# Attention on Trainium2: queries of a later head turned right behind the last key tile of the next head, and the pieces of the maxima behind them placed one behind each score

## What is computed

```python
q_pool = q.reshape(B, H, S // 2, 2, D).mean(axis=3)       # B 4, H 8, S 1152, D 64
scores = scale * np.matmul(q_pool, k.transpose(0, 1, 3, 2))
scores = scores - np.max(scores, axis=-1, keepdims=True)
attn = np.exp(scores)
attn = attn / (np.sum(attn, axis=-1, keepdims=True) + 1e-09)
return np.matmul(attn, v)
```

## Time and profile before

| | |
|---|---|
| median of 3 runs | 1168.25 us |
| the profiled execution's own time | 1168.3 us |
| its span, from first to last instruction | 1166.5 us |
| around the span | 1.8 us |
| mean granted TensorE clock | 0.992 of full speed |
| attention | from the start to about 500 us |
| PE busy | 1118.7 us, 96% of the span |
| DVE, POOL, ACT busy | 807.6, 689.0 and 620.7 us |

### The profile page before, as it was taken

One profiled execution on the slowest core, in us unless ns is written; L12 is line 12 of the kernel. 1 busy time (PEld: TensorE's weight loads), 2 busy tenths in 40 slices (PEclk: granted clock), 3 DMA queues, 4 the chain that ended last, 5 costly groups with the idle time before them and its releaser, 6 DMA issues. The chain is left out here.

```text
span 1166.5 us, 19903 instructions
## 1 busy us (share of the span) xinstructions
PE 1118.7 (96%) x7088; PEld 928.8 (80%) x7088; DVE 807.6 (69%) x1573; ACT 620.7 (53%) x1228; POOL 689.0 (59%) x694
## 2 busy tenths in 40 slices
PE   6999999999999999997998989889999999999998
PEld 5777788777877778786877777668888888888897
DVE  5788888888888888866556555675548764685554
ACT  4666666666666666546565656643334333433331
POOL 5899999998899899834333335532254333632330
PEclk9999999999999999998999999999999999999999
DMA  8211122222221111000001002332112521233121
GB/s 209 62 54 47 55 63 62 62 62 62 62 62 55 45 56 41 22 13 25 1 1 41 2 26 71 105 104 72 50 60 73 181 57 53 72 90 103 53 63 55
DMA packets 76593, 71.47 MB, mean 61 GB/s; under 512 B 11856, under 2 KB 54864, under 8 KB 76496
## 3 DMA queue, kind: packets, MB, share of 16 engines
q1 hardware_dynamic: 75888, 69.90, 19.8%
q10 hardware_dynamic: 608, 0.30, 0.1%
HBM read 60.74 MB, written 9.44 MB: 60 GB/s over the span
## 5 line engine op out<-in xcount | busy, mean ns | idle before, releaser
L653 DVE TENSOR_REDUCE part_max<-psA 128x1 f32<-128x384 f32 x465 | 250.5, 556 | 55.5 <-PE psA L388 31.9
L582 ACT ACTIVATE pT<-psA 128x576 f32<-128x576 f32 x288 | 187.8, 652 | 154.0 <-PE psA L407 144.2
L279 POOL TENSOR_TENSOR pT<-pT 128x576 f32<-128x576 f32 x157 | 222.6, 1418 | 24.0 <-ACT pT L582 1.5
L2177 DVE TENSOR_TENSOR hidden_parts<-psC,hidden_parts 128x384 f32<-128x384 f32 x168 | 91.0, 554 | 123.5 <-PE psC L2024 121.5
L388 PE MATMUL psA<-kT,qT 128*128 128x384 f32 x465 | 165.7, 378 | 1.1 <-DVE part_max L653 0.6
L421 PE MATMUL psA<-pT,v_raw 128*64 128x288 f32 x1152 | 153.8, 412 | 0.0
L1848 POOL TENSOR_TENSOR w_raw<-w_raw 128x256 f32<-128x256 f32 x24 | 18.1, 756 | 206.8 <-DMA w_raw<-in_moe_w_ch 206.6
L398 PE MATMUL psA<-qT,kT 128*128 128x288 f32 x576 | 132.3, 311 | 0.0
L407 PE MATMUL psA<-qTm,kT 128*128 128x288 f32 x576 | 123.3, 296 | 0.5 <-ACT qTm L568 0.5
L421 PEld LDWEIGHTS psA<-pT,v_raw 128*64 128x64 f32 x1152 | 77.0, 136 | 53.2 <-issue 6.4
L398 PEld LDWEIGHTS psA<-qT,kT 128*128 128x128 f32 x576 | 98.6, 189 | 18.3 <-issue 14.0
(11 more groups left out here) (196 smaller groups left out, 2631.2 us busy)
## 6 DMA issues: line engine op xcount, KB each, us to landing
w_raw<-in_moe_w_ch SPq DMA_DIRECT2D x48, 256.0 KB, 3.1
k_raw<-in_k SPq DMA_DIRECT2D x32, 288.0 KB, 3.2
v_raw<-in_v SPq DMA_DIRECT2D x32, 288.0 KB, 2.8
q_raw<-in_q SPq DMA_DIRECT2D x31, 256.0 KB, 3.3
w_even<-in_moe_w_ch SPq DMA_DIRECT2D x12, 512.0 KB, 5.0
w_odd<-in_moe_w_ch SPq DMA_DIRECT2D x12, 512.0 KB, 4.8
u_rows<-x_all SPq DMA_DIRECT2D x16, 256.0 KB, 2.0
u_even<-u_rows SPq DMA_DIRECT2D x2, 1536.0 KB, 6.8
```

The source lines that it names most:

```text
L279: nc.gpsimd.tensor_tensor(pT[:, KT, :], pT[:, KT, :], pT[:, j, :], ALU.add).then_inc(part_summed, 1)
L582: nc.scalar.activation(pT[:, j, :].rearrange("p (a c) -> p a c", a=2), scores[n % 2][:, :, 0:HALF], ACT.Exp, scale=0.5 * float(D) ** -0.5) ...
L653: nc.vector.tensor_reduce(part_max[u][:, t, c:c + 1], maxes[n % 2][:, 0:PIECE], AX.X, ALU.max).then_inc(max_freed[n % 2], 1)
L2177: nc.vector.tensor_tensor(to, session((k, n))[:, 0:W], other, ALU.add).then_inc(added, 1)
```

## The change

On PE, `turn_queries(h + 2)` moves from behind m3 to right behind the "kc" lot of head h + 1. From there on m2 goes ahead of s1 and m3 ahead of s2, where they stood behind s1 and s2. The order from s3 on is as it was. On ACT the copy of the turned queries moves from behind e2 to right behind the copies of "kc", so ahead of e1. No instruction is added, taken away or resized.

```diff
                 score(h, 0)
                 maxima(0, 2)
                 turn_keys(h + 1, "kc", [KT - 1])
-                score(h, 1)
-                maxima(2, 3)
-                score(h, 2)
-                maxima(3, 4)
                 if more2:
                     turn_queries(h + 2)
+                maxima(2, 3)
+                score(h, 1)
+                maxima(3, 4)
+                score(h, 2)
                 maxima(4, 5)
                 score(h, 3)
                 maxima(5, 6)
...
                     exponent(h, j)
                     if j == 0:
                         copy_keys(h + 1, "kc")
-                    if j == 2 and more2:
-                        copy_queries(h + 2)
+                        if more2:
+                            copy_queries(h + 2)
                     if j == 5 and more2:
                         copy_keys(h + 2, "ka")
```

## The result

The changed kernel takes 1176.56 us in the median of 5 runs (1175.32 to 1179.6), the kernel before 1168.27 us (5 runs, 1167.49 to 1171.03). The ratio is 1.0072, 95% interval 1.0056 to 1.0089: 8.3 us slower. The forecast was 1177.4, with a range of 1172.3 to 1181.0.

A forecast was written before the change was run, and what follows sets the result against it. PE and DVE were taken to bound each other by handing over pieces of the maxima. Heads 1 to 29 at 0.30 us (8.7) and head 30 at 0.36, together 9.1, on 1168.3 gave 1177.4 us; range 1172.3 to 1181.0.

The forecast's parts named there:

- m2's place: PE, top of a head: m2's weight load starts 0.05 us behind m0's reduction in either order; s1 follows m2 by 0.28.
- Three scores between m2 and m5: PE: three scores replace two scores and the transposes between m2 and m5, making m5 0.16 us later a head.
- s3 waits for e1: PE: s3 needs the score buffer e1 reads, is released at 317.68, m5 starts at 318.31; bounds nothing and 0.29 us.
- The weight load behind a waiting piece: PE, s1 behind waiting m2: its load isn't made ahead, so 0.28 us is kept; otherwise some 0.10 a head lower.
- The copy of the queries at nothing: ACT, ahead of e1: the 0.59 us copy ends 0.2 us before e1's scores are there, so it costs nothing.
- the one I priced at 0.15: Rival on ACT: transposes or copy last longer, e1 a further 0.15 us late, 0.45 a head, 1182.3 us; chance 0.06.
- Nothing given back: PE and DVE behind m5: m7 and all that follows move with m5, and no place returns the time.
- The sum: Whole attention: heads 1 to 29 lose 29 x 0.30 = 8.7 us, with head 30 together 9.1 us.
- Head 0, put at nothing: First head, running at its own start-up pace: left at no loss; one head weighs 0.3 us either way.
- the 0.36 of the forecast: Head 30, without transposes to lose: m5 would stand 2.33 us behind m2's release, not 1.97, 0.36 us more.
- lowest corner: PE: smallest loss if only the order costs, 0.06 us a head, given as 1170.5 us.
- order alone: Rival on PE: 0.16 us a head, no wait for e1 or s1's load pulled ahead, 1173.3 us; chance 0.16.

The follow-up runs named there:

- its control: Kernel before, with the exponent of tile 1 computed for the first 288 of 576 queries in heads 1 to 30: 1167.68 us, ratio 0.9992.
- second-half kernel: Kernel before with s4 ahead of m7, row sums between m7 and m8, and later pieces, scores and turn of ka rewoven: 1164.98 us, ratio 0.998.

## Why the prediction was right

Forecast 1177.4, measured 1176.56; forecast 9.1 us of loss, measured 8.3, and 8.8 in the attention of the profiled execution. By its own steps:

- *m2's place.* Forecast: 0.05 behind the end of m0's reduction in either order, s1 another 0.28 behind. Measured 0.05 and 0.28. The run with only the pieces moved shows the same place with nothing in front of it.
- *Three scores between m2 and m5.* Forecast 0.16 a head. Measured 0.15: with e1 shortened the changed kernel is at 15.49, against 15.34.
- *s3 waits for e1.* Forecast 0.13 to 0.14. Measured 0.13, by the shortened exponent and its control. This was the step that hung on 0.05 us of reckoning, and it held.
- *The weight load behind a waiting piece.* The row at m7 said that it isn't made ahead, and in the changed kernel it isn't either: s1's load starts at 321.25, 0.11 behind m2's own load (321.14), which is the one that waits, and s1 follows m2 by 0.28. The Trainium skill (TensorE: Matmul & The Clock Gate, Step-by-step: what each phase is for) speaks of weight loads that are pulled ahead of matmuls in flight. This trace doesn't contradict that; it shows that no load was made ahead of a piece that still waited.
- *The copy of the queries at nothing.* It ends at 321.84, e1 starts at 322.14, and putting it back changes nothing. Where it was in the way, with PE's old order, it cost 1.26 us a head (16.60 against 15.34). That is a later turn than the one I priced at 0.15, so that price wasn't tested.
- *Nothing given back.* m7's whole delay reaches the next head, but for some 0.02: forecast distance 15.64, measured 15.63 between the first and last head of the even part. The profile shows no other return.
- *The sum.* 9.1 against 8.3 by the medians is within what the runs scatter (the interval of the ratio is 6.5 to 10.4 us); by the attention alone it is 9.1 against 8.8. That this is so near is in part luck. By the distances of single heads, heads 1 to 29 cost 8.1 and not 8.7. Head 0, put at nothing, cost 0.27 (its distance went from 14.92 to 15.19). Head 30 cost 0.37, against the 0.36 of the forecast (15.72 to 16.09). Together that is 8.7; the 8.8 comes from rounded starts.
- *A slip.* The lowest corner of the rival "order alone" at 0.06 a head is 31 x 0.06 = 1.9 us, so 1170.2 and not 1170.5. Nothing hangs on it.

One number came out wrong behind the prediction: the expectation of the run with the early turn alone had 0.02 to 0.08 us a head, and it costs 0.21, for a score behind transposes is longer than I reckoned and m4 takes over the stop of m2. The prediction's own rows had the hint: there m4 and s3 behind the transposes took 0.77 and not 0.70. So three of the four ways to place these two things are slower than the kernel before, two with a stop at m2 and one with a stop at m4.

## What to carry to other kernels

Where two engines hand two buffers to and fro, a piece can't start before a fixed time behind the piece two places before it. Count what stands between such a pair: work that fits exactly is hidden, and less of it leaves a stop that everything queued behind it pays for. Here a short job (the transposes) took the place of a long one (a score), and the stop was the difference. An independent long job in front of a piece that waits takes the stop away, as s4 in front of m7 showed. Then look for the next release that becomes late: here it was an exponent in the changed kernel, and the other engine's sums in the kernels with s4 moved.

## What the runs showed of the hardware that I had not expected

- A wait that was fulfilled long ago isn't free on PE when the instruction stands first in the queue: m4 with two waits started 0.12 us behind the reduction that released it, with one wait 0.05.
- A score behind transposes takes 0.60 us until the next piece starts, one behind a piece 0.52. In the run with the early turn alone its second matmul starts 0.20 behind its first, where it is 0.13 in a score behind a piece. That its weight loads set the pace there is likely and not shown.
- DVE's first sum of the exponents (L674), the same instruction in every kernel, has no fixed length. In the second-half kernel over the even part (least, median and most in ns):

```profile
L674 DVE SCALAR_TENSOR_TENSOR p_sum<-pT x27: 926/1222/1547, 65.5 to 463.2; 128x576 f32<-128x576 f32 x27
```

  In the changed kernel these are 757, 974 and 1348. The traces show what its length hangs on: POOL's addition of exponents (L273 or L279) that is under way when it starts. In the head shown with that run the addition ends at 324.70 + 1.40 = 326.10 and the sum at 325.50 + 1.22 = 326.72, which is 0.62 behind it. In all 205 cases of the 13 profiles, over the even part, in which 0.15 us or more of the addition were left, the sum ended 0.61 to 0.62 us behind the addition's end, however early it had started. So the sum seems to make no headway while that addition runs, and a head in which the sum starts sooner gets a longer sum and not an earlier end. Where less than 0.05 us was left, the sum ended 0.71 us or more behind it, up to 1.38, mostly 0.61 behind the end of POOL's next instruction. This is read from the times; no run took POOL's additions away.
